# Softmax weights scaled before their transpose, V as TensorE's weights, and a second turn of lag, in a three-layer kernel on one core

## The reference

```python
# attention, for each batch (4), head (8) and chunk (24 chunks of 32)
scores = scale * np.matmul(q_c, k_full.transpose(0, 1, 3, 2))   # 32 x 64
scores = scores - np.max(scores, axis=-1, keepdims=True)
a = np.exp(scores)
a = a / (np.sum(a, axis=-1, keepdims=True) + 1e-09)
out[:, :, c_start:c_end] = np.matmul(a, v_full)                 # 32 x 64
...
x = out.transpose(0, 2, 1, 3).reshape(B * S, H * D)             # 3072 x 512
x = (x @ w_a) * (x @ w_b) @ w_out                               # 512 -> 1536 -> 512
...
h = np.maximum(x @ w1[e], 0.0)                                  # 512 -> 1024, e of 8
out += P[:, e:e + 1] * (h @ w2[e])
```

## Time and profile before

| what | value |
| --- | --- |
| median of 3 runs | 2621.83 us (2621.21 to 2624.89) |
| the profiled execution | 2617.21 us, its span 2615.5 us |
| PE busy | 2552.2 us (98% of the span), 14418 matmuls |
| PEld busy | 2101.2 us (80%) |
| POOL, DVE, ACT busy | 1640.9 us (63%), 1560.7 us (60%), 994.5 us (38%) |
| mean granted clock of TensorE | 0.996 of full speed |

### The profile page before, as it was taken

How to read it: one execution, slowest core, us unless ns; L and a number is a source line. 1 busy time by engine, 2 the same in 40 slices (tenths; PEclk the granted TensorE clock), 3 DMA queues, 4 the chain that set the end, 5 groups by cost and what they waited for, 6 DMA issues and landing times.

```text
span 2615.5 us, 38013 instructions
## 1 busy us (share of the span) xinstructions
PE 2552.2 (98%) x14418; PEld 2101.2 (80%) x14418; DVE 1560.7 (60%) x2293; ACT 994.5 (38%) x1722; POOL 1640.9 (63%) x1329
## 2 busy tenths in 40 slices
PE   7889999999999999999999999999999999999998
PEld 6678788788777888888888888888887888888887
DVE  3654544544667555555566667666666566666666
ACT  4653422322434334343343333333334333333333
POOL 2375400200477777777767777777779777777776
PEclk8999999999999999999999999999999999999999
DMA  9765533334265666666665554545555555555553
GB/s 213 164 230 215 223 151 146 145 145 165 95 263 229 254 243 229 243 256 253 241 253 206 202 220 179 224 185 199 204 194 187 207 210 205 197 202 208 188 222 117
DMA packets 190061, 530.42 MB, mean 203 GB/s; under 512 B 55544, under 2 KB 124088, under 8 KB 170680
## 3 DMA queue, kind: packets, MB, share of 16 engines
q1 hardware_dynamic: 168792, 517.43, 53.8%
q10 hardware_dynamic: 21088, 10.55, 1.6%
HBM read 367.41 MB, written 160.60 MB: 202 GB/s over the span
## 4 chain that ended last, share of the span: by engine, by line
PE 90%; DVE 4%; issue 2%; ACT 2%; POOL 1%; SPq 0%; DMA 0%; ACTq 0%; DVEq 0%; POOLq 0%
PE bank L1010 45%; PE bank L1109 22%; PE bank L1087 19%; PE bank L918 1%; PE bank L948 1%; PE bank L972 1%; DVE tmp L1734 1%; PE bank L960 0%; DVE hid L1944 0%; POOL X L749 0%; SPq L608 0%; DVE Y L1769 0%; POOL H L871 0%; PE bank L982 0%; DMA W<-w_kept 0%
## 5 line engine op out<-in xcount | busy, mean ns | idle before, releaser
L1010 PE MATMUL bank<-X,W 128*128 128x512 f32 x5550 | 1397.0, 390 | 11.8 <-DVE tmp L1731 4.3
L1010 PEld LDWEIGHTS bank<-X,W 128*128 128x128 f32 x5550 | 1038.3, 188 | 236.9 <-issue 17.3
L871 POOL TENSOR_TENSOR H<-tmp,H 128x512 fp32r<-128x512 f32 x448 | 579.6, 1307 | 285.7 <-ACT H L1550 284.4
L1109 PE MATMUL bank<-H,W2n 128*128 128x512 f32 x2688 | 682.4, 389 | 5.6 <-DVE Y L1789 2.1
L1789 DVE TENSOR_TENSOR Y<-Y,bank 128x512 f32<-128x512 f32 x752 | 496.8, 682 | 262.5 <-PE bank L1109 262.5
L1109 PEld LDWEIGHTS bank<-H,W2n 128*128 128x128 f32 x2688 | 503.8, 188 | 113.2 <-POOL H L871 6.3
L1550 ACT ACTIVATE H<-tmp 128x512 fp32r<-128x512 f32 x448 | 276.9, 630 | 464.9 <-DVE tmp L1819 238.9
L1087 PE MATMUL bank<-W,hid 128*128 128x512 f32 x1536 | 385.5, 390 | 1.8 <-DVE Y L1766 1.0
L1087 PEld LDWEIGHTS bank<-W,hid 128*128 128x128 f32 x1536 | 287.8, 188 | 63.5 <-issue 3.4
L749 POOL TENSOR_TENSOR X<-Y,X 128x1024 fp32r<-128x1024 f32 x30 | 79.9, 2670 | 368.6 <-ACT X L1346 368.6
L1766 DVE SCALAR_TENSOR_TENSOR Y<-bank,gate,Y 128x512 f32<-128x512 f32 x224 | 167.2, 747 | 165.8 <-PE bank L1087 164.7
(11 more groups left out here) (121 smaller groups left out, 2135.9 us busy)
## 6 DMA issues: line engine op xcount, KB each, us to landing
W<-w_kept SPq DMA_DIRECT2D x88, 1792.0 KB, 11.9
W2n<-w2n_kept SPq DMA_DIRECT2D x64, 1536.0 KB, 8.5
w_kept<-W SPq DMA_DIRECT2D x44, 1792.0 KB, 8.1
raw<-in_moe_w_dram SPq DMA_DIRECT2D x64, 512.0 KB, 4.4
w2n_kept<-W SPq DMA_DIRECT2D x32, 1024.0 KB, 7.9
w2n_kept<-tmp SPq DMA_DIRECT2D x64, 512.0 KB, 8.1
W2n<-w2n_kept SPq DMA_DIRECT2D x64, 256.0 KB, 3.0
W<-w_kept SPq DMA_DIRECT2D x12, 1024.0 KB, 9.1
```

Of the source, the lines that this page charges most:

```text
L871: nc.gpsimd.tensor_tensor(H[:, pos, 1], hidden_at(k, pos), H[:, pos, 0].bitcast(F32), ALU.subtract).then_inc(h_lo, 1)
L1010: last = nc.tensor.matmul(into[:, :], W1[:, c % 2, ws, w_slot, kc, :], X[:, pos, xs, kc, :], start=(start and kc == 0 and n == 0), stop=(k ...
L1109: last = nc.tensor.matmul(b_half[pair][half][:, :], W2n[k % 2][:, a, blk, half * P:(half + 1) * P], H[:, h, b, :], start=(q in (0, 5) and ...
```

## The change

- `quotients(r)` now multiplies the exponentials in `Pr` themselves by `rsum`, in one operation of 128x512, before the transpose.
- In `weigh_v(r)` the two sides are swapped: V (64 keys x 64 columns) is the weights, P (32 queries) the moving side. The result comes with features on the partitions, so `transpose_o`, `On` and the bank `b_ot` go, and `x_quad(r)` copies from `b_o[r % 2]`. Both f of a quad now write to the same bank, in different partitions.
- `transpose_p` and `weigh_v` of quad r run in turn r + 2 instead of r + 1. `copy_pt` and `x_quad` on ACT move with them. Behind turn 23 there are now two quads to finish, between the first products.
- `Vw` has 4 slots instead of 3, so that the memory rows are loaded for four quads of each batch (2 DMAs more in each batch, 8 in all), and `load_v(3)` stands ahead of `put_rows` of batches 1 to 3.
- The small tiles `nmax`, `esum`, `rsum` are placed elsewhere, and some waits go: POOL's and PE's for `a_on` of the last quad, ACT's for `a_sum`.

```diff
-    VS = 3
+    VS = 4
...
         def loads_v(r):
-            return sum((12, 10, 10, 8, 8, 10)[i % G] for i in range(r % VS, r + 1, VS))
+            return sum((12, 10, 10, 10, 8, 10)[i % G] for i in range(r % VS, r + 1, VS))
...
             load_v(2)
+            load_v(3)
             for b in range(1, B):
                 put_rows(b)
...
             def transpose_p(r):
-                pe.wait_ge(a_exp, r + 1)
-                if edge(r):
-                    pe.wait_ge(a_pad, edges_to(r))
+                pe.wait_ge(a_on, r + 1)
...
             def weigh_v(r):
                 pe.wait_ge(a_ptc, r + 1)
                 pe.wait_ge(s_v[r % VS], 16 * loads_v(r))
-                if r > 0:
-                    pe.wait_ge(a_on, 2 * r)
+                if r > 1:
+                    pe.wait_ge(a_x, r - 1)
                 for hp in range(HP):
                     for c in range(4):
                         for f in range(2):
-                            rows = slice(64 * f, 64 * f + 64)
-                            last = nc.tensor.matmul(b_o[f][32 * c:32 * c + 32, hp * HD:(hp + 1) * HD],
-                                                    PT[rows, hp, c * CHUNK:(c + 1) * CHUNK],
-                                                    Vw[rows, r % VS, c, hp, :], start=True, stop=True)
+                            rows, at = slice(64 * f, 64 * f + 64), hp * P + c * CHUNK
+                            last = nc.tensor.matmul(b_o[r % 2][rows, at:at + CHUNK], Vw[rows, r % VS, c, hp, :],
+                                                    PT[rows, hp, c * CHUNK:(c + 1) * CHUNK], start=True, stop=True)
                 last.then_inc(a_o, 1)
-
-            def transpose_o(r):
-                pe.wait_ge(a_on, 2 * r + 2)
-                if r > 0:
-                    pe.wait_ge(a_x, r)
-                for hp in range(HP):
-                    last = nc.tensor.transpose(b_ot[:, hp * P:(hp + 1) * P], On[:, hp, :, :], ident[:, :])
-                last.then_inc(a_ot, 1)
...
             for r in range(R):
                 scores(r)
-                if r > 0:
-                    transpose_p(r - 1)
                 if r > 1:
-                    transpose_o(r - 2)
+                    transpose_p(r - 2)
                 for unit in QUAD_UNITS[r][:1]:
                     transposed(unit)
-                if r > 0:
-                    weigh_v(r - 1)
+                if r > 1:
+                    weigh_v(r - 2)
                 for unit in QUAD_UNITS[r][1:]:
                     transposed(unit)
...
             def x_quad(r):
-                act.wait_ge(a_ot, r + 1)
+                act.wait_ge(a_o, r + 1)
...
             def quotients(r):
-                dve.wait_ge(a_o, r + 1)
                 dve.wait_ge(a_rs, r + 1)
-                if r > 0:
-                    dve.wait_ge(a_ot, r)
-                for f in range(2):
-                    nc.vector.tensor_tensor(On[:, :, f, :],
-                                            b_o[f][:, 0:HP * HD].rearrange("p (j n) -> p j n", j=HP),
-                                            rsum[:, :, f:f + 1].to_broadcast([P, HP, HD]),
-                                            ALU.mult).then_inc(a_on, 1)
+                p = Pr[:, r % 2].rearrange("p h f n -> p (h f) n")
+                by = rsum[:, :, :].rearrange("p h f -> p (h f)").unsqueeze(2).to_broadcast([P, HEADS, KEYS])
+                nc.vector.tensor_tensor(p, p, by, ALU.mult).then_inc(a_on, 1)
```

More of the change, by code:

```diff
@@ L132, in build @@
             PT = sb("PT", [P, HP, P], F32, first)
-            On = sb("On", [P, HP, 2, HD], F32, first)
             Df = sb("Df", [P, HP, 2, KEYS], F32, first)
             Pr = sb("Pr", [P, 2, HP, 2, KEYS], F32, first)
-            nmax = sb("nmax", [P, 2, HP], F32, first)
-            esum = sb("esum", [P, HP, 2, 2], F32, first)
-            rsum = sb("rsum", [P, HP, 2], F32, first)
         hid0 = sb("hid0", [P, 2, 2, 2, TB], F32R)
@@ L144, in build @@
             KT1 = sb("KT1", [P, HP, KCOLS], F32, first)
+            nmax = sb("nmax", [P, 2, HP], F32, first)
+            esum = sb("esum", [P, HP, 2, 2], F32, first)
+            rsum = sb("rsum", [P, HP, 2], F32, first)
         hid1 = sb("hid1", [P, 2, 2, 2, TB], F32R)
@@ L167, in build @@
         bank = [ctx.enter_context(nc.psum_tensor(f"bank{i}", [P, 512], F32)) for i in range(8)]
-        b_s, b_t, b_pt, b_o, b_ot = bank[0:2], bank[2:4], bank[4], bank[5:7], bank[7]
+        b_s, b_t, b_pt, b_o, b_warm = bank[0:2], bank[2:4], bank[4], bank[5:7], bank[7]
         b_down = bank[3:6]
@@ L194, in build @@
         a_sum = sem("a_sum")
+        a_den = sem("a_den")
+        a_rs = sem("a_rs")
+        a_on = sem("a_on")
         a_pt = sem("a_pt")
@@ L198, in build @@
         a_o = sem("a_o")
[L199 to L202, removed]
         a_x = sem("a_x")
@@ L719, in down_lo @@
                     pool.wait_ge(a_pt, R)
-                    pool.wait_ge(a_on, 2 * R)
                 nc.gpsimd.tensor_tensor(W2[w % 2][:, 1, :], raw[:, item_w2(w) % 2, :], W2[w % 2][:, 0, :].bitcast(F32),
@@ L970, in weigh_v @@
                         for f in range(2):
-                            rows = slice(64 * f, 64 * f + 64)
-                            last = nc.tensor.matmul(b_o[f][32 * c:32 * c + 32, hp * HD:(hp + 1) * HD],
-                                                    PT[rows, hp, c * CHUNK:(c + 1) * CHUNK],
-                                                    Vw[rows, r % VS, c, hp, :], start=True, stop=True)
+                            rows, at = slice(64 * f, 64 * f + 64), hp * P + c * CHUNK
+                            last = nc.tensor.matmul(b_o[r % 2][rows, at:at + CHUNK], Vw[rows, r % VS, c, hp, :],
+                                                    PT[rows, hp, c * CHUNK:(c + 1) * CHUNK], start=True, stop=True)
                 last.then_inc(a_o, 1)
-            def transpose_o(r):
-                pe.wait_ge(a_on, 2 * r + 2)
-                if r > 0:
-                    pe.wait_ge(a_x, r)
-                for hp in range(HP):
-                    last = nc.tensor.transpose(b_ot[:, hp * P:(hp + 1) * P], On[:, hp, :, :], ident[:, :])
-                last.then_inc(a_ot, 1)
             pe.wait_ge(s_zero, 2)
             for i in range(WARM):
-                nc.tensor.matmul(b_ot[:, 0:P], ident[:, :], ident[:, :], start=True, stop=True)
+                nc.tensor.matmul(b_warm[:, 0:P], ident[:, :], ident[:, :], start=True, stop=True)
             for unit in FIRST_UNITS:
@@ L1076, in down @@
                 elif i == 2:
-                    pe.wait_ge(a_on, 2 * R)
+                    pe.wait_ge(a_x, R)
                 else:
@@ L1165, in total @@
                                  stop=True).then_inc(g_total, 1)
+            transpose_p(R - 2)
             pe.wait_ge(a_sub, 2 * R)
             up(0, 0, 0)
+            weigh_v(R - 2)
+            up(0, 1, 0)
             transpose_p(R - 1)
-            transpose_o(R - 2)
-            up(0, 1, 0)
+            up(0, 2, 0)
             weigh_v(R - 1)
-            up(0, 2, 0)
-            transpose_o(R - 1)
             for pos in range(3, NP):
@@ L1287, in exps @@
                     act.wait_ge(a_pt, r - 1)
-                    act.wait_ge(a_sum, r - 1)
                 d, p = (t.rearrange("p h f n -> p (h f) n") for t in (Df[:, :, :, :], Pr[:, r % 2]))
@@ L1302, in x_quad @@
             def x_quad(r):
-                act.wait_ge(a_ot, r + 1)
+                act.wait_ge(a_o, r + 1)
                 nc.scalar.activation(Y[:, :, r * QUAD:(r + 1) * QUAD],
-                                     b_ot[:, :].rearrange("p (c n) -> p c n", c=KC), ACT.Copy).then_inc(a_x, 1)
+                                     b_o[r % 2][:, :].rearrange("p (c n) -> p c n", c=KC), ACT.Copy).then_inc(a_x, 1)
             def up_hi(c, pieces=(0, 1, 2, 3)):
@@ L1321, in down_hi @@
                 if w == 0:
-                    act.wait_ge(a_pt, R)
-                    act.wait_ge(a_sum, R)
+                    act.wait_ge(a_o, R)
                 elif w >= 2:
@@ L1353, in _ @@
             for r in range(R):
-                if r > 0:
-                    copy_pt(r - 1)
                 if r > 1:
-                    x_quad(r - 2)
+                    copy_pt(r - 2)
+                if r > 2:
+                    x_quad(r - 3)
                 exps(r)
@@ L1377, in _ @@
                     up_hi(1, (2, 3))
+            copy_pt(R - 2)
+            x_quad(R - 3)
             copy_pt(R - 1)
```

1 line of the change is left out of this document (removed).

## The result

| what | before | after |
| --- | --- | --- |
| median, run side by side, 6 runs each | 2623.36 us (2620.26 to 2626.6) | 2633.41 us (2628.29 to 2636.34) |
| ratio to before | | 1.0038, 95% interval 1.0027 to 1.0049 |
| the profiled execution, its span | 2617.21, 2615.5 us | 2628.29, 2626.6 us |
| PE busy over the span | 2552.2 us | 2567.3 us |
| start of `up(0, 3)` in the profiled execution | 150.98 us | 160.51 us |

The change makes the kernel 10.0 us slower, 0.38%, and its interval lies clear of 1. I had forecast 2629 us, +7 to the profiled execution.

A forecast was written before the change was run, and what follows sets the result against it. PE's own work and SP's V stream bound the attention up to `up(0, 3)`, the later lane deciding. PE's lane: 21.6 - 2.7 - 7.5 + 2 - 7 = +6.4, taken as +7: profiled 2624, median 2629 us, range 2622 to 2642.

The forecast's parts named there:

- V's lane: SP's stream of V loads: 8 added DMAs cost 3.6 us, putting `up(0, 3)` at 153.8 us, +2.8; chance 0.30.
- the block, 24 quads: PE's product with V as weights: 1.75 us a block instead of 0.85, +0.9 us a quad, +21.6 us.
- transposes of the result: Removed from PE: 0.1 us gained in each of 17 turns, two times 0.44 in the tail, together -2.7 us.
- waits for V: PE's waits ahead of `weigh_v`: one more turn of lag frees PE of them, -7.5 us.
- low clock: PE in the first 150.7 us: a seventh of the time at 1.2 GHz, where added work counts double, +2 us.
- waits for instructions: PE's waits inside blocks of alike matmuls, about 16 us: longer turns shrink them, -7 us.
- P's transpose waiting for DVE: DVE's scaling ahead of `transpose_p`: hidden by the rest of the turn, 4 us, so put at nothing.
- V stays the bound: Rival: waits shrink more or PE's gaps absorb the work, so V's lane holds, +2.8 us, 2625 us; chance 0.30.
- The block doesn't grow: Rival: 64-column weights cost no more than 32-column ones in PE's product, +1 us, 2623 us; chance 0.07.
- The two halves get in each other's way: Rival: halves writing one bank run serially, block 3.5 us, +47, 2669 us; 0.13 shared with partial serialisation or a 2.0 us block.
- a block of 2.0 us and waits that don't shrink: PE's product block at 2.0 us, waits for instructions kept: +19.4 us; within the 0.13 shared with serialised halves.
- Faster: Rival: instructions come sooner on SP and PE, both lanes shorten, V's lane at -12.2 us, 2610 us; chance 0.05.

The follow-up runs named there:

- tail: Changed kernel with DVE's operand_sum(0, 0, 4) behind the last quad's scaling and POOL's last clear between pieces of up_lo(1): 2633.93 us, 1.0038 to before.
- more DMAs: Changed kernel with 16 more DMAs of memory rows on SP's queue: 2632.0 us, 1.0042; the same added to the kernel before: 2625.29 us, 1.0006.
- three slots: Changed kernel with three slots for V, which takes the 8 added DMAs away again: 2633.71 us, 1.004 to before.
- one pair scaled: Changed kernel with DVE's scaling done for one of four head pairs, the others left unscaled: 2629.88 us, 1.0024 to before.
- the lag alone: Kernel before with transpose_p, weigh_v and transpose_o one turn later, two rsum buffers, P still the weights, three V slots: 2620.32 us, repeated 2620.2, both 0.9991.
- narrow weights: Changed kernel with 32 of V's 64 columns as weights, the other half of the output's features left out: 2622.73 us, 0.9998 to before.
- two banks: Changed kernel with the product's halves f = 0 and f = 1 in different banks, each copied by its own operation: one run, 2654.13 us.
- product doubled: Kernel before with each of weigh_v's matmuls issued twice, 128 instead of 64 in a block: 2665.71 us, 1.0165 to before.

## Why the prediction came out right

The direction, the place and the lane were right: PE's work decides, V's lane does not, and the added work is the product's block. Term by term, in the profiled executions:

| term of PE's lane | predicted | measured | from |
| --- | --- | --- | --- |
| the block, 24 quads | +21.6 | +27.7 | the two groups, 50.3 - 22.6 |
| transposes of the result | -2.7 | -7.4 | PE's other busy time, 14.8 - 27.7 = -12.9, and the waits for P's copy, 9.0 - 3.5 |
| waits for V | -7.5 | -8.1 | none left in front of a whole block |
| low clock | +2 | within the rows above | 21 us at 1.2 GHz before, 13 after: half of the 8 is about -4 |
| waits for instructions | -7 | -6.3 | 16.4 and 10.1 us |
| P's transpose waiting for DVE | 0 | +2.4 | the group of L957 |
| waits for the copies of K and Q | no term | +1.2 | 5.4 and 6.6 us |
| sum | +6.4 | +9.5 | `up(0, 3)` +9.5 |

The sum is exact by its making: busy time and waits are all that PE's lane has. Luck has a part in the +6.4. The block came out 6 us dearer than I took it, and the clock, in this pair of executions, some 6 us better than my +2. Either miss alone would have been as large as the forecast.

**The block is the term that was mis-sized.** "L929 is nearest in both, so I take 1.75 us": that is 64 loads at 27 ns. The loads came at 29 ns, which is 1.81 us from the first to the last, and that is not yet the block: what stands behind it starts another 0.18 us later, 1.99 us. The 0.85 us it was compared with was taken from start to start and held that end already. The bound of 2.0 us from the line through L933 has the right size for another reason: it came from 31 ns a load, and the loads take 29; the 0.18 us behind them make up the rest.

**The transposes of the result.** "Together -2.7 us" took L957 to L971 as 1.34 us, and so it is in 17 of the 24 quads. The transposes stood in PE's lane in full, though, and their going shows as less busy time and 5.5 us more of waits for P's copy. Part of the -7.4 is the clock: at 1.2 GHz L960 to L972 took 2.75 us in two quads before, against 1.45.

**DVE's scaling was put at nothing, and the cover was not there in the last turns.** Its mean is 931 ns against the 919 I took from L1734, so the size was right on average; the last one took 1.72. But "what hides the scaling is the rest of the turn, 4 us" counted the usual turn. In the last ones DVE also has the next layer's operands, and P's transpose waits 2.4 us. With a quarter of the scaling these waits are 0.2 us.

**The waits for instructions** shrank by about what was said. The four profiled variants with the same 64-column block on one bank (tail, more DMAs, three slots, one pair scaled) have 9.4, 6.3, 8.8 and 4.2 us. The kernel before and the lag alone have 16.4, 15.8 and 22.2. The narrow weights, with the changed kernel's instructions and nearly the short block, have 13.1. So they are fewer where each 256 instructions keep PE busy longer, which fits "the fetch less the work"; how much of it is that, no run shows apart.

**V's lane** was put at +2.8 us by 3.6 us of added issue. SP's last V load is at 146.36 us, 1.2 later than in the earlier trace rows: eight DMAs in a stream of unsteady pace did not show in full. It plays no part, since the last block starts at 158.53.

**The rivals.** "V stays the bound" is out: no wait for V is left, and 16 more DMAs on the changed kernel change nothing. "The block doesn't grow" is out by the rows. "The two halves get in each other's way" is out in its strong form by the block of 1.99 us and by the two banks. Its weak form, "a block of 2.0 us and waits that don't shrink", +19.4 us, was half right: the block is 2.0 us, but the waits did shrink. "Faster" is out: of the waits for instructions 10 us stay, and 13 us at the lower clock.

What stays open: the clock. Up to `up(0, 3)` the profiled variants of the changed kernel with one bank have mean clocks from 0.87 to 0.96, and behind it all profiled executions take 2466 to 2468 us, so the spread between them arises in the attention. The profiled execution of the changed kernel is its fastest run, that of the kernel before is faster than all its six, and the -4 belongs to this pair. The mean granted clock of its six runs is 0.9932, that of 23 runs of the kernel before 0.9943, which makes 2 x 0.0011 x 2625 = 6 us more at 1.2 GHz, or 3 us of time, the other way. So how the +10.0 of the medians divides between the terms isn't settled, though it agrees with the +9.5 of `up(0, 3)`.

The lowest median of the study is the lag alone, 2.7 us or 0.1% below before, with an interval that just reaches 1.

## What to carry to other kernels

Swapping the sides of a small product to save a transpose trades moving columns for weight columns, and the second can be the dearer ones when a block alternates between few tiles of the array: here 96 transposes went, some of whose time was cover for a copy, and 1,536 weight loads became 29 ns instead of 10. Count a block from its start to the start of what follows, on both sides of the comparison. When waits stand in the middle of alike instructions, number PE's instructions: if the waits fall on every 256th, as here, they are hardly waits for data, and more instructions mean more of them. And don't book a wait that is taken away as time gained: the lag alone took most of V's late waits, and PE's unnamed waits in all were 24 to 27 us in either.

## What the hardware showed beyond that

- Two halves of the array that write to one PSUM bank run as fast as with two banks, in a block whose weight loads come every 29 ns: 2.06 us a block either way.
- A weight load costs 0.82 ns a column on its own tile (57 and 31 ns for 64 and 32 columns), and loads of different tiles overlap: every 10 ns with eight tiles of 32 columns, 16 ns with two of 32, 29 ns with two of 64.
- PE's waits in the middle of a block, with no semaphore there, stand at every 256th of its instructions, in all 13 profiled executions. They come to 16 us in the first 150 before, 16 and 22 with the lag alone, 10 with the longer block, and 44 us in the first 200 with the product doubled.
